# Delta-rule attention with two expert layers on one core: the second pair's diagonal blocks turned by TensorE, and the first pair's products laid in another order

## What is computed

```python
def _attn_ref(q, k, v, beta):          # batch 4, heads 8, seq 768, head_dim 48
    k_n = k / (norm(k) + 1e-06)
    state = zeros(B, H, D, D)
    for t in range(S):
        y[t] = q[t] @ state
        state += beta[t] * outer(k_n[t], v[t] - k_n[t] @ state)
...
x = y as rows                                             # 3072 x 384
h = maximum(maximum(x @ w1, x @ w2), x @ w3); x = h @ w_out        # 768 wide
# then: noisy top-2 gate over 8 experts, each token's two experts
out[tok] += gate * (maximum(x[tok] @ w1[e], 0.0) @ w2[e])          # 1024 wide
```

## Time and profile before

| | us |
|---|---|
| median of 3 runs | 1025.73 (1025.57 to 1025.75) |
| the profiled execution | 1025.56 |
| its span in the trace | 1023.8 |
| PE busy in the span | 997.9 (97%) |
| DVE, ACT, POOL busy | 721.6, 469.7, 214.8 |
| mean granted TensorE clock | 0.988 of full speed |

### The profile page before, as it was taken

The page is one execution under the profiler, slowest core; times in us unless marked ns, Lnnn a source line. Parts: engine busy times, 40 slices in busy tenths (PEclk is TensorE's granted clock), DMA queues, the critical chain, the costliest instruction groups (busy, mean ns, idle before and its releaser), DMA issues.

```text
span 1023.8 us, 25726 instructions
## 1 busy us (share of the span) xinstructions
PE 997.9 (97%) x10425; PEld 929.1 (91%) x10425; DVE 721.6 (70%) x1701; ACT 469.7 (46%) x700; POOL 214.8 (21%) x229
## 2 busy tenths in 40 slices
PE   8899999999999999999999999999999999999995
PEld 7888898898888888888899999999999999999995
DVE  7988795893884786543569677778677686776772
ACT  4542345226325325233363546546465465654651
POOL 0464310210120130121315221212211112212111
PEclk8899999999999999999999999999999999999998
DMA  9540320420430330116656625234352526526221
GB/s 306 129 109 2 94 53 23 129 61 3 126 85 3 78 93 2 57 42 217 220 188 179 186 43 169 47 88 122 53 156 47 170 39 172 163 55 169 40 30 24
DMA packets 71190, 101.68 MB, mean 99 GB/s; under 512 B 28608, under 2 KB 59584, under 8 KB 70720
## 3 DMA queue, kind: packets, MB, share of 16 engines
q1 hardware_dynamic: 59024, 78.10, 25.4%
q0 software_dynamic: 10992, 20.70, 10.5%
q10 hardware_dynamic: 1088, 1.65, 0.5%
HBM read 136.98 MB, written 29.51 MB: 163 GB/s over the span
## 4 chain that ended last, share of the span: by engine, by line
PE 92%; DVE 3%; ACT 3%; issue 2%; POOLq 0%; POOL 0%; ACTq 0%; DVEq 0%
PE ps L1895 43%; PE ps L2061 20%; PE ps L1944 8%; PE ps L1744 3%; PE ps L2072 3%; PE ps L1874 2%; PE ps L1850 2%; PE ps L1725 2%; PE ps L1862 2%; PE ps L1960 2%; PE ps L1784 1%; DVE prod L1176 1%; DVE x L1180 1%; PE ps L1830 1%; ACT solve L862 1%
## 5 line engine op out<-in xcount | busy, mean ns | idle before, releaser
L1895 PE MATMUL ps<-xr,wr_in 128*128 128x512 f32 x972 | 235.8, 396 | 0.3 <-ACT xr L888 0.3
L1895 PEld LDWEIGHTS ps<-xr,wr_in 128*128 128x128 f32 x972 | 178.6, 188 | 39.6 <-DVE wr_in L1298 0.5
L1895 PE MATMUL ps<-xbT,w1r 128*128 128x256 f32 x1728 | 211.6, 283 | 0.6
L1895 PEld LDWEIGHTS ps<-xbT,w1r 128*128 128x128 f32 x1728 | 209.7, 192 | 2.5 <-issue 2.1
L2061 PE MATMUL ps<-w2r,hbT 128*128 128x384 f32 x1152 | 205.9, 336 | 0.0
L2061 PEld LDWEIGHTS ps<-w2r,hbT 128*128 128x128 f32 x1152 | 198.9, 188 | 0.0
L754 POOL DMA_INDIRECT out_rows<-yb,idx x55 | 91.5, 1664 | 374.8 <-DVE yb L1524 289.1
L965 ACT ACTIVATE hbT<-ps 128x512 fp32r<-128x512 f32 x96 | 57.3, 597 | 166.6 <-PE ps L1895 163.4
L1336 DVE TENSOR_TENSOR w1r<-w1s,w1r 128x768 fp32r<-128x768 f32 x124 | 117.3, 956 | 17.2 <-ACT w1r L949 15.1
L949 ACT CAST w1r<-w1s 128x768 fp32r<-128x768 f32 x124 | 101.2, 828 | 24.8 <-DMA w1s<-in_we 24.8
L1336 DVE TENSOR_TENSOR w2r<-w2s,w2r 128x768 fp32r<-128x768 f32 x124 | 110.2, 950 | 2.0 <-ACT w2r L953 2.0
(11 more groups left out here) (232 smaller groups left out, 1125.6 us busy)
## 6 DMA issues: line engine op xcount, KB each, us to landing
w1s<-in_we SPq DMA_DIRECT2D x31, 1536.0 KB
w2s<-in_we SPq DMA_DIRECT2D x31, 1536.0 KB
xb<-rows SPq DMA_DIRECT2D x24, 402.0 KB
kv_s<-in_kv SPq DMA_DIRECT2D x24, 384.0 KB, 3.7
k_s<-in_k SPq DMA_DIRECT2D x12, 512.0 KB, 4.0
joint<-in_q SPq DMA_DIRECT2D x24, 256.0 KB
out_rows<-padrow SPq DMA_DIRECT2D x13, 384.0 KB, 4.3
w_in<-in_w_blocks SPq DMA_DIRECT2D x3, 1152.0 KB, 9.7
```

The lines of the kernel that those rows point to most:

```text
L1895: mm = pe.matmul(dst, w, m, start=(opens and n == 0), stop=(closes and n == len(todo) - 1))
```

## The change

1. **Turning by TensorE.** The second pair's diagonal blocks are no longer turned by DVE (`rows_of(1)` is gone) but by 128 matmuls with the identity, 32x32 each (`blocks_to_rows`, after `first_k_q`), then copied by ACT (`blocks_in_rows`) over `diag`, which takes the place of `ag` for that pair. `roots(1)` and `norms(1)` come earlier.
2. **Keep-warms.** 3 for each step from 16 to 29 instead of 2 from 18, and 8 as before: 50 instead of 32. The 22 other keep-warm products of the prologue are gone.
3. **Order.** `first_low(1)` ahead of `first_corner(0)`; `outputs`, the second state step and the products of `u` in two halves of heads; half of chunk 0's outputs behind `k_state_and_q(1)`; half of the second state step ahead of `to_xT`, half behind. Copies of `u` and `y` go by quarters.
4. **POOL** takes 15 steps of the second pair's inverse instead of 12 and does `weights_low(0)` just before them; DVE's 16 remaining steps are spread over products 3 to 9.

```diff
+        row_blocks = [ag, diag] + [ag] * (CP - 2)
...
-        POOL_STEPS = {1: 12, 2: 11}
+        POOL_STEPS = {1: 15, 2: 11}
...
+        def half_turns(one, n):
+            for i in range(HP):
+                one(1 - n, HP + i)
+                last = one(n, i)
+            return last
...
             if t == 0 and n == 1:
-                return early + (Q - 1 - early) * min(i + 1, low) // low
+                return early + (Q - 1 - early) * min(max(i - 2, 0), low - 3) // (low - 3)
...
# POOL
-            weights_low(0)
             zero_x(1)
             pool.wait_ge(s_xz, 2)
             first_pT(1)
             pool.wait_ge(p_low, 1)
             pool.wait_ge(s_off, 4)
             nc.gpsimd.tensor_copy(off[:], off_early).then_inc(s_off_moved, 1)
+            weights_low(0)
             pool_base(1)
...
# ACT
+            def blocks_in_rows():
+                act.wait_ge(p_rows, 1)
+                nc.scalar.copy(row_blocks[1][:].rearrange("p (k i) b -> p k (i b)", k=2), ps[:, E_BANKS:E_BANKS + 2]
+                               ).then_inc(s_gb, 1)
...
-            weights_high(0, 4)
+            folded_gate()
+            weights_high(0, 2)
             first_k_q()
-            folded_gate()
+            blocks_in_rows()
+            roots(1)
+            weights_high(2, 4)
             first_low(0)
             first_solve(0, 0)
             first_solve(0, 1)
             first_corner(0)
-            roots(1)
             first_low(1)
             first_solve(1, 0)
             first_solve(1, 1)
             u_out(0)
             first_corner(1)
             first_state()
-            y_out(0)
+            first_y_half(0)
             out_weights_high()
-            u_out(1)
+            first_y_half(1)
+            first_u_half()
+            second_u_half()
+            second_y_half(0)
+            second_y_half(1)
+            x_high(0)
             weights_high(4, FT)
-            y_out(1)
-            x_high(0)
...
# DVE
             transposed_columns_of(0)
-            rows_of(1)
+            norms(1, (0, 1))
             first_corner_half(0)
-            norms(1, (0,))
-            u_half(0)
+            norms(1, (2,))
+            first_u()
             first_corner_half(1)
-            norms(1, (1,))
             first_state()
-            norms(1, (2,))
             scaled_v(1)
-            weights_low(1, (0, 1))
+            weights_low(1, (0,))
             r_out(1)
-            pT_out(1, (0,))
-            weights_low(1, (2,))
-            u_half(1)
-            pT_out(1, (1,))
+            pT_out(1)
+            second_u_half()
+            weights_low(1, (1, 2))
+            second_y_half(0)
+            second_y_half(1)
             norm_columns(1)
+            weights_low(2, (0,))
+            x_low(0)
+            weights_low(2, (1, 2))
             state_out(1)
-            y_half(1)
-            weights_low(2)
-            x_low(0)
...
# PE
+            def blocks_to_rows():
+                pe.wait_ge(s_diag, 4)
+                pe.wait_ge(s_const, N_CONST)
+                for i in range(Q):
+                    for g in range(4):
+                        rows = slice(g * Q, g * Q + Q)
+                        mm = pe.matmul(ps[rows, E_BANKS + i // (Q // 2), i % (Q // 2) * Q:(i % (Q // 2) + 1) * Q],
+                                       diag[rows, :, i], ident[rows, rows], start=True, stop=True)
+                mm.then_inc(p_rows, 1)
...
-                pe.wait_ge(s_y, 4 * cp + 4)
+                pe.wait_ge(s_y, 4 * cp + 8)
...
                     pe.wait_ge(s_xh, 2)
-                    pe.wait_ge(s_state, 3)
...
             first_k_q()
-            for k in range(18, Q - 2):
-                keep_warm(E_BANKS + 1, 2, k)
-            keep_warm(E_BANKS + 1, 8, Q - 2)
+            blocks_to_rows()
+            for k in range(16, Q - 2):
+                keep_warm(C_BANKS, 3, k)
+            keep_warm(C_BANKS, 8, Q - 2)
             first_low(0)
-            keep_warm(C_BANKS, 3)
+            first_low(1)
             first_corner(0)
-            first_low(1)
             solve_u(0)
             first_corner(1)
             state_step(0)
-            outputs(0)
+            first_outputs(0)
             k_state_and_q(1)
-            keep_warm(H_BANKS, 3)
+            first_outputs(1)
             solve_u(1)
-            keep_warm(H_BANKS, 3)
-            state_step(1)
-            outputs(1)
+            second_outputs(0)
+            second_outputs(1)
+            state_step(1, (0,))
             pe.wait_ge(s_const, N_CONST)
-            keep_warm(C_BANKS, 4)
             to_xT(0, 0)
             to_xT(0, 1)
-            keep_warm(C_BANKS, 4)
+            state_step(1, (1,))
```

More of the change, by code:

```diff
@@ L372, in by_bank_pair, with half_places @@
             return ap.rearrange("p (g a) t -> p g a t", g=2)
-        def turns(one):
[L376 to L382, removed]
+        def half_turns(one, n):
[3 more added lines that the diff above has]
+            return last
+        def turns(one):
+            half_turns(one, 0)
+            return half_turns(one, 1)
+        def half_places(n):
+            return ((n, 0), (1 - n, 1))
         def gram_banks(c):
@@ L868, in u_out, with first_u_half, second_u_half, first_y_half @@
                 act.wait_ge(p_u, c + 1)
[L869 removed]
+                for h_ in range(2 if c else 1):
                     nc.scalar.copy(by_bank_pair(state_u(c, h_, tokens(h_))), token_products(h_)).then_inc(s_u, 1)
+            def first_u_half():
+                act.wait_ge(p_u_half, 1)
+                for h_, g in half_places(0):
+                    nc.scalar.copy(u_half_rows(1, h_, g), half_products(D_BANKS, h_, g)).then_inc(s_u_half, 1)
+            def second_u_half():
+                act.wait_ge(p_u, 2)
+                h_, g = half_places(1)[0]
+                nc.scalar.copy(u_half_rows(1, h_, g), half_products(D_BANKS, h_, g)).then_inc(s_u, 1)
+            def first_y_half(n):
+                act.wait_ge(p_y if n else p_y_half, 1)
+                for h_, g in half_places(n):
+                    nc.scalar.copy(y_half_rows(0, h_, g), half_products(H_BANKS if n else D_BANKS, h_, g)).then_inc(s_y, 1)
+            def second_y_half(n):
+                act.wait_ge(p_y if n else p_y_half, 2)
+                h_, g = half_places(n)[0]
+                nc.scalar.copy(y_half_rows(1, h_, g), half_products(D_BANKS, h_, g)).then_inc(s_y, 1)
             def y_out(c):
                 act.wait_ge(p_y, c + 1)
[L874 to L876 removed]
+                act.wait_ge(p_xT, c // 2 * 2)
+                for h_ in range(2):
                     nc.scalar.copy(y_rows(c, h_), token_products(h_)).then_inc(s_y, 1)
@@ L1124, in norms @@
                 G = 7
-                squares = ag[:].rearrange("p i k -> p (i k)")[:, ::Q + 1]
+                blocks = row_blocks[cp][:]
+                squares = blocks.rearrange("p i k -> p (i k)")[:, ::Q + 1]
                 if 0 in parts:
@@ L1851, in one, with state_step @@
                                      solve[rows, c % 2 * PAIRS + a], kv_s[rows, 1, a], start=True, stop=True)
[L1852 to L1856, removed]
+                if c == 1:
+                    half_turns(one, 0).then_inc(p_u_half, 1)
+                    half_turns(one, 1).then_inc(p_u, 1)
+                else:
+                    turns(one).then_inc(p_u, 1)
+            def state_step(c, halves=(0, 1)):
+                if 0 in halves:
+                    pe.wait_ge(s_u, 2 * c + 2)
+                    pe.wait_ge(s_k, c * 16 + 16)
                 if c > 1:
                     pe.wait_ge(s_pT, c + 2)
-                first = C_BANKS if c > 1 else H_BANKS
+                first = C_BANKS if c else H_BANKS
                 def one(h, a):
@@ L1863, in one, with outputs_of, outputs, first_outputs @@
                                      kv_s[tokens(h), 0, a], joint[c % 2][h][tokens(h), a, 0:D], start=True, stop=True)
[L1864 to L1870, removed]
+                for n in halves:
+                    mm = half_turns(one, n)
+                if 1 in halves:
+                    mm.then_inc(p_s, 1)
+            def outputs_of(c, n, first):
                 def one(h, a):
                     rows = slice(0, P if h else L + D)
-                    return pe.matmul(ps[tokens(h), D_BANKS + a // HP, a % HP * D:a % HP * D + D],
+                    return pe.matmul(ps[tokens(h), first + a // HP, a % HP * D:a % HP * D + D],
                                      joint[c % 2][h][rows, a, D:], joint[c % 2][h][rows, a, 0:D], start=True, stop=True)
-                turns(one).then_inc(p_y, 1)
+                return half_turns(one, n)
+            def outputs(c):
+                outputs_of(c, 0, D_BANKS)
+                outputs_of(c, 1, D_BANKS).then_inc(p_y, 1)
+            def first_outputs(n):
+                if n == 0:
+                    pe.wait_ge(s_state, 1)
+                    pe.wait_ge(s_pT, 2)
```

(8 more changed lines are left out.)

48 lines of the change are left out of this document (34 added, 14 removed).

## The result

| | before | changed |
|---|---|---|
| median, us | 1025.67 (1025.57 to 1025.75) | 1031.72 (1030.49 to 1033.01) |
| profiled execution | 1025.56 | 1030.99 |

Ratio 1.0062, 95% interval [1.0049, 1.0075]: the change is slower by 6 us. The forecast was slower by 3.0, and its range ended at 1031.2: the time lies 0.5 us above it.

The account below looks back on a forecast made before the run. PE's work bounds the kernel, so the stream's start decides: turning to 35.9, keep-warms to 47.4, plus 23.1 gives 70.5, 3.0 us later than 67.46. So 1025.56 + 3.0 = 1028.6 us, range 1023.8 to 1031.2.

Parts of the forecast that it names:

- What bounds the kernel: PE's own work sets the end once the stream runs; the kernel's time moves with the stream's start, 67.46 us before.
- the hidden terms: Work on POOL, DVE and SP beside PE's queue: forecast to cost nothing, or up to 1 us if DVE's slack is gone.
- The turning with two fetch pauses: PE's 128 matmuls after `first_k_q`: stalls after about 106 and 233 of 256 records, end at 35.9 us (bounds 31.9 to 37.0).
- Rival 1: Instruction fetch does not delay the turning, which ends at 33.6 us; kernel 1024.9 us. Chance 0.25.
- The price of a record: In the turning on PE: 256 records taken to cost 4.3 us at full clock, 7.7 us at half clock.
- rival 2: Turning over four row groups at once: 8.4 ns a record, 15 at half clock; kernel faster, 1021.9 us. Chance 0.10.
- The keep-warms: 50 back to back on PE ahead of `first_low(0)`: 11.0 us plus 0.5 for half clock, so it starts at 47.4 us.
- The upper bound, 2.0: Most extra time, in us, for the 50 keep-warms: the case where four us of them go at half clock.
- From `first_low` to the stream, 23.1: PE's prologue: durations sum to 22.2 us plus a stall of 0.9, against 28.6 before; the stream starts at 70.5.
- the stall of 0.9: One instruction-fetch stall in the prologue, placed in `first_outputs(0)`: 0.9 us, bounds 0 and 2.2.
- rival 3: Clock falls in the prologue, no keep-warms between `first_low` and the stream: 2 us more per stretch, 1030.6 to 1032.6. Chance 0.08.
- Range: The forecast's own span, 1027.0 to 1031.3 us; the overall range, 1023.8 to 1031.2, takes in rival 1 too.

Follow-up runs that it names:

- e5: The changed kernel once more, nothing altered, beside the kernel before: 1033.17 us, ratio to before 1.0085.
- e13: The changed kernel again, unaltered, in the group that compares shares side by side: 1026.86 us, ratio to before 1.0068.
- e9: Changed kernel, its 50 keep-warms replaced: 12 among the turning's matmuls, 6 behind the last step, 3 each side of `first_corner(0)`; DVE's corner copy earlier: 1022.14 us, ratio 1.0029.
- e8: The changed kernel with 16 unread 32x32 matmuls (32 records) added ahead of `first_k_q`: one run, 1032.34 us.
- e1: The changed kernel with the 32 keep-warms of before ahead of `first_low` instead of 50: 1024.95 us, ratio to before 1.006.
- e12: The changed kernel with 3 keep-warms added before and 3 behind `first_corner(0)`: 1025.50 us, ratio to before 1.0059.
- e2: The changed kernel with only the 8 keep-warms behind the last step instead of 50: 1021.89 us, ratio to before 1.0026.
- e14: e1 again, 32 keep-warms instead of 50, now beside the changed kernel: 1024.62 us, ratio to before 1.0052.

## Why the prediction was wrong

The sum against three profiles of the changed kernel (us; PE's timeline):

| | forecast | first profile | e5 | e13 |
|---|---|---|---|---|
| the turning is over | 35.9 | 35.9 | 35.6 | 35.3 |
| the 50 keep-warms | 11.5 | 14.0 | 12.8 | 13.7 |
| from `first_low(0)` to the stream | 23.1 | 22.9 | 26.8 | 25.3 |
| the stream starts | 70.5 | 72.8 | 75.2 | 74.3 |

- **What bounds the kernel**: right. Nothing changed in the stream (5.3 us at its start, 5.4 at the end), and the hidden terms (POOL's 15 steps, DVE's base, the loads) cost nothing.
- **The turning with two fetch pauses, end at 35.9**: right, 35.95 (and 35.3 to 36.9 in the other profiles, e9 with its keep-warms in between apart). e8 shows the mechanism. Rival 1 falls: fetches aren't hidden here, in disagreement with the Trainium skill's "mostly hidden" (Runtime: NRT & Kernel Launch, "Instruction fetch mechanics"). The price of a record was wrong and did no harm: 7.7 us were reckoned for the records at half clock, but the first 105 took 1.67 us at 0.50, 16 ns each. That is the 15 ns of rival 2. Products that go between two row groups take 29 ns at 0.50 (`first_corner(1)` in e5, 64 records from 55.93 to 57.77), those with one group 54 (e8). So going round four groups did pay at half clock; at full clock it didn't (128 records in 2.03 us in e1 as well, 1.0 us of it at 1.00, where two groups take 16.7 ns). The time of rival 2 did not come, since the fetches and not the records set the end.
- **The keep-warms**: the term that failed. "I take 0.5, nearer to 0, since PE has been busy for 12 us by then": they took 14.05 us against 11.5, and 12.8 to 13.8 in e5, e8, e12 and e13. The clock was at half when they began and rose 3.1 to 5.6 us into them. Having been busy was the wrong ground: 4.1 of the 12 us were the turning's own pauses; in e9 PE had work for 18 us and the clock stayed at 0.50; in e1, e2 and e14 it rose in the turning and was down again before the keep-warms. Whether it is the turning's small products or its pauses that leave the clock at half stays open: e9 takes the pauses out, but puts other work in. The upper bound, 2.0, was too small in the first profile, where the extra is 3.0. It was taken from one rise in the trace before, four us into the keep-warms. The term was 2.5 us short, and the profiled execution lies 2.4 above the forecast.
- **From `first_low` to the stream, 23.1**: 22.9 in the first profile, right in size and partly by luck: the stall of 0.9 that it placed in `first_outputs(0)` did not come, and waits of 0.2 to 0.3 us for DVE and ACT stand in its place. And it is so only where the clock holds. In e5 and e13 it falls at 52 and 54 us, and the stretch takes 26.8 and 25.3. I gave that (rival 3) a chance of 0.08, on the ground that PE goes from 44 to 50 us without keep-warms before and keeps 1.00; I overlooked that three keep-warms stood at 40 us. The profiled execution has no such fall, so this second term is no part of its 2.4 us. The median lies 0.7 above it; e5 and e13 make the fall the likely cause, but no profile of the other three runs is there to show it.
- **Range**: its upper end had 2.0 for the clock in the keep-warms and nothing for the clock in the prologue. (By its own terms it runs from 1027.2 to 1031.2, not from 1027.0 to 1031.3.)

## What to carry to other kernels

Keep-warm products ahead of a dependent chain are a queue: count them in time at the lower clock, and against the moment at which the chain's data are ready. Before taking out the ones between short products, check the clock over several executions. Here, with 32 or more ahead of the chain, six between its products were worth more than they cost, while 42 of the 50 ahead of it cost 5.1 us more than they gave. And small products have a second price, their instructions: see where the fetch pauses of the trace before fall, and count records to the next one.

## What the runs showed of the hardware

- PE's instructions come in blocks; with small products (16 to 17 ns a record) PE ran out of them about every 127 records. From the end of the turning's first pause to the end of its second it took 3.7 to 4.8 us in ten profiles, and 6.5 in e5. 32 records inserted ahead moved both pauses by 32.
- The granted clock stayed at 0.50 through 18 us of PE work without a pause (e9: 32x32 products with a keep-warm behind every 8 or 12). At 28.6 us in e1 it rose while 32x32 products ran. Behind the turning it rose 2.8 to 5.6 us into the keep-warms where there were 32 or 50 of them.
- A record of a 32x32 product takes 16 ns at 0.50 and at 1.00 when the products go round four row groups. With two groups it takes 17 ns at 1.00 and 29 at 0.50, with one 54 at 0.50. A 64x48 product's 64 records take 2.07 against 3.65 us.
- The same kernel took 1019.3 us on one chip and 1025.0 on another, a difference nearly as large as the loss of the changed kernel.
